# A table of powers spread over the partitions straight from SBUF, in place of a way through DRAM

## The reference

```python
def _attn_ref(q, k, v, lam):            # q, k, v: (2, 8, 768, 64), lam: (8,)
    block = 64
    rel = pos[:, None] - pos[None, :]
    Dmask = np.where(rel >= 0, lam[:, None, None] ** rel[None, :, :], 0.0)
    lam_pow = lam[:, None, None] ** (pos[None, :, None] + 1)
    lam_block = lam ** block
    for b in range(nb):
        intra = np.einsum('bhic,bhjc->bhij', qb, kb) * Dmask[None]
        intra = np.einsum('bhij,bhjd->bhid', intra, vb)
        inter = np.einsum('bhid,bhde->bhie', qb * lam_pow[None], kv_state)
        out[:, :, sl] = intra + inter
        rev_pow = lam[:, None, None] ** (block - 1 - pos[None, :, None])
        kb_dec = kb * rev_pow[None]
        kv_state = lam_block[None, :, None, None] * kv_state + np.einsum('bhsd,bhse->bhde', kb_dec, vb)
```

## Time and profile before

| | us |
|---|---|
| median of 3 runs | 488.47 |
| lowest and highest of them | 488.31, 488.76 |
| the profiled execution, own time | 488.76 |
| its span, first to last instruction | 486.9 |
| busy in the span: PE | 459.2 (94%) |
| busy in the span: DVE, ACT, POOL | 260.4, 210.9, 92.6 |

### The profile page before, as it was taken

The page is one execution under the profiler, slowest core; times in us unless marked ns, Lnnn a source line. Parts: engine busy times, 40 slices in busy tenths (PEclk is TensorE's granted clock), DMA queues, the critical chain, the costliest instruction groups (busy, mean ns, idle before and its releaser), DMA issues.

```text
span 486.9 us, 7685 instructions
## 1 busy us (share of the span) xinstructions
PE 459.2 (94%) x2635; PEld 391.4 (80%) x2636; DVE 260.4 (53%) x421; ACT 210.9 (43%) x337; POOL 92.6 (19%) x137
## 2 busy tenths in 40 slices
PE   7899997699999999999999996599999999999997
PEld 7788886577878787878788884498899889889985
DVE  2677885355564737473829194495444544616401
ACT  1133331073645545464636373487244533714400
POOL 2436752522221222222222221000000000000000
PEclk9899999799999999999999999599999999999999
DMA  6999881048392929393867500700010000010001
GB/s 218 406 398 329 327 313 66 22 139 299 113 311 99 309 96 296 115 284 144 261 256 239 192 29 27 268 1 0 22 46 0 22 22 22 0 43 22 0 23 43
DMA packets 28460, 70.87 MB, mean 146 GB/s; under 512 B 3154, under 2 KB 4178, under 8 KB 28436
## 3 DMA queue, kind: packets, MB, share of 16 engines
q1 hardware_dynamic: 22946, 57.95, 33.8%
q0 software_dynamic: 2800, 9.18, 5.7%
q10 hardware_dynamic: 2690, 3.44, 2.0%
HBM read 59.53 MB, written 11.02 MB: 145 GB/s over the span
## 4 chain that ended last, share of the span: by engine, by line
PE 80%; DVE 9%; issue 3%; DMA 3%; POOL 2%; DVEq 1%; ACT 0%; SPq 0%; POOLq 0%; ACTq 0%
PE bank L1024 21%; PE bank L1026 20%; PE bank L1025 20%; DVE wl L790 5%; PE bank L954 3%; PE bank L943 2%; PE bank L930 2%; PE bank L964 2%; PE bank L1048 2%; PE bank L972 2%; PE bank L1034 2%; POOL slot_row L408 1%; PE bank L918 1%; PE bank L979 1%; DVE hl L784 1%
## 5 line engine op out<-in xcount | busy, mean ns | idle before, releaser
L790 DVE TENSOR_TENSOR wl<-raw,wh 128x1024 fp32r<-128x1024 f32 x64 | 74.6, 1218 | 0.0
L509 ACT ACTIVATE wh<-raw 128x1024 fp32r<-128x1024 f32 x64 | 64.1, 1054 | 0.0
L784 DVE TENSOR_TENSOR hl<-bank,hh 128x512 fp32r<-128x512 f32 x32 | 22.1, 690 | 64.0 <-ACT hh L505 64.0
L1024 PE MATMUL bank<-wh,hh 128*128 128x512 f32 x128 | 52.8, 412 | 2.6 <-DVE hl L784 1.6
L1024 PE MATMUL bank<-wh,xh 128*128 128x512 f32 x128 | 51.4, 402 | 1.7 <-DVE xl L780 1.7
L1026 PE MATMUL bank<-wh,hl 128*128 128x512 f32 x128 | 50.2, 392 | 0.0
L1026 PE MATMUL bank<-wh,xl 128*128 128x512 f32 x128 | 50.0, 391 | 0.0
L1025 PE MATMUL bank<-wl,hh 128*128 128x512 f32 x128 | 49.8, 389 | 0.0
L1025 PE MATMUL bank<-wl,xh 128*128 128x512 f32 x128 | 49.8, 389 | 0.0
L500 ACT ACTIVATE h_sb<-bank 128x512 f32<-128x512 f32 x32 | 19.1, 596 | 64.8 <-PE bank L1026 64.8
L1024 PE MATMUL bank<-xkh,wh 128*128 128x384 f32 x128 | 43.0, 336 | 0.3 <-DVE xkl L856 0.3
(11 more groups left out here) (159 smaller groups left out, 894.2 us busy)
## 6 DMA issues: line engine op xcount, KB each, us to landing
raw<-in_w_dram SPq DMA_DIRECT2D x64, 512.0 KB, 8.0
qk_sb<-in_qk_dram SPq DMA_DIRECT2D x12, 512.0 KB, 7.0
kv_sb<-in_kv_dram SPq DMA_DIRECT2D x12, 512.0 KB, 6.1
x_dram<-keep ACTq DMA_DIRECT2D x12, 256.0 KB, 6.2
keep<-y_dram SPq DMA_DIRECT2D x12, 256.0 KB, 5.3
out_dram<-o_sb SPq DMA_DIRECT2D x12, 256.0 KB, 2.0
raw<-in_w_k_dram SPq DMA_DIRECT2D x4, 512.0 KB
raw<-in_w_v_dram SPq DMA_DIRECT2D x4, 512.0 KB
```

The lines of the kernel that those rows point to most:

```text
L509: act.activation(parts[1 - p][0][:, c, :], raw[:, c, :], ACT.Copy).then_inc(s["part_h"], 1)
L784: dve.tensor_tensor(hl[:, 4 * g:4 * g + 4, :], by(psT[g][:, :], 4), hh[:, 4 * g:4 * g + 4, :].bitcast(F32), ALU.subtract).then_inc(s["hl_d ...
L790: dve.tensor_tensor(parts[1 - p][1][:, c, :], raw[:, c, :], parts[1 - p][0][:, c, :].bitcast(F32), ALU.subtract).then_inc(s["part_l"], 1)
L1024: pe.matmul(ps, lhsT=a_high, rhs=b_high, start=start, stop=False)
```

## The change

`decay_rows` no longer goes through DRAM. For each of the four pairs it issues one DMA that reads the 128 overlapping stretches of 512 B from the one partition of `pw` in SBUF and writes them to the 128 partitions of `decay` (64 KB). The 4 KB writes to `powers_dram`, the tensor itself and the wait between the two DMAs are gone. SP and ACT thus issue four DMAs each where there were two, and `decay_in` is awaited at 128 in place of 32. The load of chunk 1 (q and k, and k and v) moves from ahead of the decay on SP to behind it.

```diff
-        def decay_rows(eng, a):
-
-            eng.wait_ge(s["powers_done"], 1)
-            eng.dma_start(powers_dram[a:a + 1, :], flat(pw[a * DH:a * DH + 1, :, :])).then_inc(powers_out[a], 16)
-            eng.wait_ge(powers_out[a], 16)
-            powers = bass.AP(powers_dram.tensor, a * HP * 2 * P, [[1, P], [2 * P, HP], [1, P]])
-            eng.dma_start(decay[:, a, :, :], powers).then_inc(s["decay_in"], 16)
+        def decay_rows(eng, a, pair):
+
+            at = a * DH * HP * 2 * P + pair * 2 * P
+            powers = bass.AP(pw.tensor, at, [[HP * 2 * P, 1], [1, P], [1, P]])
+            eng.dma_start(decay[:, a, pair, :], powers).then_inc(s["decay_in"], 16)
...
-            for t in range(2):
-                load_qk(t)
-                load_kv(t)
-            decay_rows(sp, 0)
-            for t in range(2, RING):
+            load_qk(0)
+            load_kv(0)
+            sp.wait_ge(s["powers_done"], 1)
+            for pair in range(HP):
+                decay_rows(sp, 0, pair)
+            for t in range(1, RING):
                 load_qk(t)
                 load_kv(t)
...
-            pool.wait_ge(s["decay_in"], 32)
+            pool.wait_ge(s["decay_in"], 128)
...
-            decay_rows(act, 1)
+            act.wait_ge(s["powers_done"], 1)
+            for pair in range(HP):
+                decay_rows(act, 1, pair)
...
-            dve.wait_ge(s["decay_in"], 32)
+            dve.wait_ge(s["decay_in"], 128)
```

More of the change, by code:

```diff
@@ L70, in sem @@
             return ctx.enter_context(nc.semaphore(name))
-        powers_dram = nc.dram_tensor("powers_dram", [2, HP * 2 * P], F32).ap()
         x_dram = nc.dram_tensor("x_dram", [N + P, D], F32).ap()
@@ L208, in mixer_kernel @@
         raw0_in = [sem(f"s_raw0_in{i}") for i in range(CH)]
-        powers_out = [sem(f"s_powers_out{i}") for i in range(2)]
         o_out = [sem(f"s_o_out{i}") for i in range(3)]
```

## The result

| | before | changed |
|---|---|---|
| median | 488.62 us (4 runs) | 496.63 us (4 runs) |
| lowest and highest | 488.31, 490.55 | 495.94, 497.08 |
| profiled execution, its own time | 488.76 | 496.07 |
| its span | 486.9 | 494.3 |

The ratio of changed to before is 1.0154, with a 95% interval of 1.0132 to 1.0177: the change costs 1.5%, 6.5 to 8.7 us of 488.6. In the profiled executions the span grew by 7.4 us.

A forecast was written before the change was run, and what follows sets the result against it. Bound by the decay's way to PE's first `update`; decay packets 6.58 to 18.4 us, chunk 1's load landed 20.1, then 2.08 + 1.89 + 1.02 put the mark at 25.1, 7.0 us later: 495.5 us, range 484.7 to 499.0.

The forecast's parts named there:

- What bounds the kernel: Start of the kernel: the decay's way, 5.52 to 13.09 us, bounds it; each us PE's first `update` moves shifts the whole.
- What goes, and the first packet at 6.58 us: Decay path: DRAM write and wait vanish, 3.0 us; decay DMA issued at 5.52 us, first packet 1.06 us later.
- The issues cost nothing: SP and ACT queues: three more issues each, 0.40 us apiece, run beside the first DMA's traffic, adding nothing to the decay.
- One source partition gives one way's share, 11.8 us a half: Decay read: each half limited to one of 16 ways into SBUF, 26.6 GB/s; 11.8 us, middle of 9.85 and 13.8.
- The allowance for the pieces: Decay read: 512 pieces through one way at 27 ns each would take 13.8 us, against 9.85 us by bytes.
- the 100 that I had named as a sign: Decay read on SP's queue: packets of over 100 ns would show that the source partition limits.
- The load behind it, 1.28 us: SP's queue: chunk 1's q and k follow the decay's packets, 1.28 us more, landing at 20.1 us, and hold `scores(1)`.
- the sum: Forecast timeline to the start of `scores(2)`: decay packets end 18.4 us, landing 18.8, load 20.1, mark 25.1 in place of 18.06.
- The clock: PE after its gap: `scores(1)` 2.08 and `update(0)` 1.89 us at low clock, then `within_chunk(0)` 1.02 us at full clock.
- Rival 1: Decay read: source partition doesn't matter, needing 87 GB/s; mark 3.5 us early, 485.0 us; chance 0.23.
- Rival 2: Decay read: a partition gives more than one way's share; 3.9 to 6.5 us, total 487.5 to 490.5 us; chance 0.07.
- Rival 3: Decay read: one-partition source confines each DMA to one engine; mark 23 us late, about 512 us; 0.04 with anything beyond.

## Why the prediction was right

The forecast was 7.0 us and 495.5 us; measured were 7.78 us at the mark and a ratio that makes 7.5 us, 496.63 us in the median. Step by step:

- **What bounds the kernel.** Right: PE's start moved the whole, with the attention's end late by the same 7.78 us as the mark.
- **What goes, and the first packet at 6.58 us.** Right: traffic began at about 6.7 us.
- **The issues cost nothing.** Wrong as put: SP's four took 5.81 us and not 1.6, and q and k of chunk 1 were issued at 11.38 and not 7.15 us. It probably did no harm, since that load's packets had to wait for SP's half anyway.
- **One source partition gives one way's share, 11.8 us a half.** The mechanism was right for SP's half, and the runs with partitions 0, 1 and 4 as sources show it; for ACT's half the width of partition 64 was not tested by itself. The size was too high: a half took 10.4 and 10.2 us, nearer to the lower end of 9.85. The allowance for the pieces was right in kind, as 256 B pieces took 12.8 us, but too large for 512 B. SP's packets took 168 ns, over the 100 that I had named as a sign.
- **The load behind it, 1.28 us.** Too low. SP's half landed at 17.4 us (18.8 in the sum) and the load at 19.72 us, 2.3 us later in place of 1.3. Until 18.8 us ACT's half, which had started 1.9 us after SP's, was still under way on the same engines, a term that the sum did not have; that it is the cause is likely and not tested. This error and the one before nearly cancel, which is luck: `scores(1)` started at 19.86 us, 20.1 forecast.
- **The clock.** Mis-sized by 1.0 us: I let the clock come back in time for `within_chunk(0)`, but it took 1.91 us and not 1.02, and `update(0)` 2.00 us and not 1.89. The view by stretch of the changed kernel (the same columns as in the earlier trace rows):

```profile
19.86:21.93 2.07, 2.07 (x17) 1.85 (x17) 0.76 (x2) 0.00 (x0) 1.11 (x2) 0.50 1.00 358
21.93:23.94 2.01, 2.01 (x11) 1.79 (x12) 1.29 (x2) 0.00 (x0) 1.18 (x2) 0.50 1.03 422
23.94:25.84 1.90, 1.90 (x18) 1.57 (x18) 1.68 (x3) 0.00 (x0) 1.05 (x1) 0.53 1.02 388
25.84:31.42 5.58, 5.58 (x63) 5.00 (x62) 3.59 (x7) 1.20 (x2) 1.60 (x1) 1.00 1.03 413
```

The granted clock is about 0.5 (1.2 GHz) for all three groups, 6.0 us after a gap of 10.47 us, where before it was 3.8 us after 2.72 us, and 1.00 (2.4 GHz) from the mark on. This 1.0 us, less the 0.24 us by which `scores(1)` was early, is the whole of the difference between 7.0 and 7.78 us. In other runs of the same place it came back sooner: with partition 4 as source `within_chunk(0)` took 1.29 us, with the smaller pieces 1.02 us. So the point is not fixed, and such a term should carry 1 us either way.

- **Rival 1, the source doesn't matter.** Fell: 26 GB/s against the 87 it needed. **Rival 2** too: it needed more than 40 GB/s. **Rival 3, one engine each.** Fell by the row of 7 to 8 us above: SP's half alone kept 0.66 of 16 engines busy, so more than ten took part.

The gain that the change was worth if the source were free, 3.5 us in the working of rival 1, was never tested, since no run here reads a decay from SBUF at full rate. That SBUF as a source is not slow in itself is shown only in part, by the 145 GB/s from several groups.

## What to carry to other kernels

Bytes from partition 0 of SBUF, or from 0 and 1 together, left at 24 to 27 GB/s with over ten DMA engines at work, from one queue or from two; 64 KB cost some 2.6 us. A detour through DRAM put 1.5 to 3.0 us in front of the read here, and it is the quicker way when the narrow source adds more than that. When a table is the same in many partitions, read different parts of it from different groups: 0 and 4, and 0, 4, 8, 12 beside 64, 68, 72, 76, worked here; other distances were not tried. When a wait on the first work of TensorE can't be shortened, fill it: here 20 small transposes were worth 0.3% and cost two lines.

## What the runs showed of the hardware beyond this

- A DMA issue is not always 0.4 us. Behind the slow source, single issues on SP took 2.05 and 2.47 us in the changed kernel, where the first two took 0.57 and 0.59. With both halves from partition 0, at half the rate, the load of chunk 1 took 5.14 us just to issue, and whatever stands behind it in SP's program waits too:

```profile
14.82 5.14 SPq L265 DMA_DIRECT2D qk_sb<-in_qk_dram  x1
20.00 5.15 SPq L268 DMA_DIRECT2D kv_sb<-in_kv_dram  x1
```

- The reads of 512 B start at any multiple of 4 bytes, and yet one source gave 24 to 27 GB/s, near the 26.6 that loads have per engine. With 256 B the rate was about a fifth lower (20.5 GB/s for SP's half).
